# One core, delta-rule attention and two expert layers: beta is applied to the solved values instead of to the keys, with new written-out orders for the attention stage

## What is computed

```
k_n = k / (norm(k) + 1e-06)
for t in range(S):
    y[t]  = q[t] @ state
    v_old = state^T k_n[t]
    state = state + beta[t] * outer(k_n[t], v[t] - v_old)
x = reshape(y)                                   # 3072 x 384
h = x @ w_in;  x = (h * tanh(softplus(h))) @ w_out      # d_ff 2048
P = 8 rounds of row and column normalising of exp(x @ w_gate - max)
out = sum over e of P[:, e] * (relu(x @ w1[e]) @ w2[e]) # 8 experts, 1024 wide
```

## Time and profile before

| | us |
|---|---|
| median of 3 runs | 2375.93 |
| lowest, highest | 2375.30, 2376.21 |
| the profiled execution, its own time | 2375.96 |
| its span, first to last instruction | 2374.0 |
| attention, to the last product of wave 11 on PE | about 403.6 of the span |

### The profile page before, as it was taken

The page is one execution under the profiler, slowest core; times in us unless marked ns, Lnnn a source line. Parts: engine busy times, 40 slices in busy tenths (PEclk is TensorE's granted clock), DMA queues, the critical chain, the costliest instruction groups (busy, mean ns, idle before and its releaser), DMA issues.

```text
span 2374.0 us, 38713 instructions
## 1 busy us (share of the span) xinstructions
PE 2339.5 (99%) x15984; PEld 1962.5 (83%) x15984; DVE 1271.0 (54%) x2322; ACT 848.3 (36%) x1887; POOL 421.5 (18%) x344
## 2 busy tenths in 40 slices
PE   6999999999999999999999999999999999999999
PEld 5899998888888788888888888888888888888887
DVE  6888878977777564433333433434333334334344
ACT  4888887756666311111111111111111111111111
...
GB/s 85 60 58 60 50 34 50 59 1 0 0 0 27 35 1 51 45 14 45 9 49 45 14 45 9 49 45 14 45 9 54 40 14 49 5 54 40 18 35 68
DMA packets 101152, 82.28 MB, mean 35 GB/s; under 512 B 75120, under 2 KB 82032, under 8 KB 99056
## 3 DMA queue, kind: packets, MB, share of 16 engines
...
q10 hardware_dynamic: 144, 0.66, 0.1%
...
## 4 chain that ended last, share of the span: by engine, by line
PE 95%; DVE 2%; POOL 1%; issue 0%; ACT 0%; DMA 0%; DVEq 0%; POOLq 0%
PE ex_h L142 47%; PE ex_y L142 45%; PE ex_logits L142 2%; DVE at_gram L480 1%; DVE at_X L524 1%; PE ex_y L581 0%; PE ex_logits L581 0%; POOL at_NT L388 0%; DVE at_norm L475 0%; POOL at_Z L394 0%; DMA at_k_in<-k 0%; DVE at_R L486 0%; ACT at_Z L443 0%; POOL at_bk L356 0%; POOL at_bk L363 0%
## 5 line engine op out<-in xcount | busy, mean ns | idle before, releaser
L1320 DVE SCALAR_TENSOR_TENSOR ex_r_lo<-ex_h,ex_r_hi 128x512 fp32r<-128x512 f32 x384 | 265.1, 690 | 929.5 <-ACT ex_r_hi L1199 929.1
L1199 ACT ACTIVATE ex_r_hi<-ex_h 128x512 fp32r<-128x512 f32 x384 | 229.8, 598 | 1285.0 <-PE ex_h L142 1285.0
L142 PE MATMUL ex_h<-x_lo,ex_w_hi 128*128 128x512 f32 x1152 | 448.1, 389 | 0.0
L142 PE MATMUL ex_h<-x_hi,ex_w_hi 128*128 128x512 f32 x1152 | 448.1, 389 | 0.0
L142 PE MATMUL ex_y<-ex_r_hi,ex_w_lo 128*128 128x512 f32 x1152 | 448.1, 389 | 0.0
L142 PE MATMUL ex_y<-ex_r_hi,ex_w_hi 128*128 128x512 f32 x1152 | 448.1, 389 | 0.0
L142 PE MATMUL ex_y<-ex_r_lo,ex_w_hi 128*128 128x512 f32 x1152 | 448.1, 389 | 0.0
L142 PE MATMUL ex_h<-x_hi,ex_w_lo 128*128 128x512 f32 x1152 | 448.1, 389 | 0.0
L1149 POOL TENSOR_TENSOR ex_w_lo<-ex_stage,ex_w_hi 128x512 fp32r<-128x512 f32 x90 | 115.7, 1287 | 1675.3 <-ACT ex_w_hi L1181 1637.1
L142 PEld LDWEIGHTS ex_h<-x_hi,ex_w_hi 128*128 128x128 f32 x1152 | 216.2, 188 | 45.0 <-issue 0.2
L142 PEld LDWEIGHTS ex_h<-x_hi,ex_w_lo 128*128 128x128 f32 x1152 | 216.2, 188 | 45.0
...
## 6 DMA issues: line engine op xcount, KB each, us to landing
...
```

What stands on the lines that cost most here:

```text
L142: return nc.tensor.matmul(out, lhsT, rhs, start=start, stop=stop)
L1199: nc.scalar.activation(r[0][:, j, :], h_bank[j][:], ACT.Relu).then_inc(hi_ready, 1)
L1320: nc.vector.scalar_tensor_tensor(out=r[1][:, j, :], in0=h_bank[j][:], scalar=0.0, in1=r[0][:, j, :].bitcast(F32), op0=ALU.max, op1=ALU.sub ...
```

## The change

- No `bk`, `bv`, `kbT`: the keys are scaled by the norm alone. `gram` applies beta to the half that becomes A, row by row, and becomes three instructions: two of 128x128 with beta as scalar (L512) and one of 128x256 (L514). `U` multiplies by beta as it copies. `R` subtracts from the plain values, and in the first chunk there is no `R`: `B2` reads the values as loaded. `inv` loses its product with beta.
- `F1` transposes 4 pairs of heads of `kn` in one step for two groups, so there are 2 steps of 4 transposes per wave instead of 4, and 2 copies on ACT.
- The squares and the scaling of wave 0 are each cut in two halves of 8 heads, `sqh.0` and `knh.1` on POOL, `sqh.1` and `knh.0` on DVE. `NT.0`, `NT.3` and `ZZ.2` of wave 0 move from POOL to DVE.
- POOL clears the state; the masks are loaded by SP in two parts, the first 4 behind the keys of wave 0.
- PE first does 12 products of 128x256 of a cleared tile (`WARM_UP`), whose result is not used.
- New order tables; the head now holds waves 0 and 1, the rounds run for r = 2 to 10, and `h1` (three products of the dense layer) stands behind all attention products in the last table.

The core of the diff (tables cut to a line):

```diff
 ATTENTION_ROUND = {
     "PE": (
-        "T5.0@-1 Z5.1@-1 F1.3:3 T5.2@-1 Z5.0@-1 X5.3@-1 res.1@-1 Z5.2@-1 res.0@-1 T5.3@-1 res.2@-1 corr.1@-1 "
+        "res.1@-1 X5.3@-1 Z5.2@-1 res.0@-1 T5.3@-1 corr.1@-1 res.2@-1 Z5.3@-1 corr.0@-1 F2.3:13 corr.2@-1 H.1 "
...
+FIRST_ROUND = 2
+WARM_UP = 12
...
-        for r in range(1, NW - 1):
+        for r in range(FIRST_ROUND, NW - 1):
...
     def pool_program(pool):
+        nc.gpsimd.memset(state[:], 0.0).then_inc(zeroed, 1)
...
-            if kind == "bk":
-                pool.wait_ge(rbeta, n + 1)
-                scaled_by(bk[w][:, :, 0:D], k_in[w][:], norm[w][:, 4, :])
-            if kind == "bv":
...
+            if kind == "sqh":
+                pool.wait_ge(loaded_k[w], 16 * (c + 1))
+                nc.gpsimd.tensor_tensor(square[:, HALF[g]], k_in[w][:, HALF[g]], k_in[w][:, HALF[g]], ALU.mult).then_inc(squared, 1)
...
+            if kind == "knh":
+                pool.wait_ge(rnorm, n + 1)
+                nc.gpsimd.tensor_tensor(kn[w][:, HALF[g], 0:D], k_in[w][:, HALF[g]], by_norm(n)[:, HALF[g]],
+                                        ALU.mult).then_inc(scaled, 1)
...
     def dve_program(dve, fill):
+        nc.vector.memset(U[0][:], 0.0).then_inc(blank, 1)
...
-                nc.vector.tensor_tensor(norm[w][:, 4, :], norm[w][:, 3, :], beta_of(n), ALU.mult).then_inc(rbeta, 1)
...
-                nc.vector.tensor_tensor(gram[w][g][:, b], O_bank[i][:].rearrange("p (i a t) -> p i a t", i=2, a=2),
-                                        nupper_upper.unsqueeze(2).to_broadcast([P, 2, 2, P]),
-                                        ALU.mult).then_inc(O_drained[i], 1)
+                for a in range(2):
+                    head = 4 * g + 2 * a + b
+                    nc.vector.scalar_tensor_tensor(out=gram[w][g][:, b, 0, a, :], in0=O_bank[i][:, a * P:(a + 1) * P],
+                                                   scalar=beta_of(n)[:, head:head + 1], in1=nupper, op0=ALU.mult, op1=ALU.mult)
+                nc.vector.tensor_tensor(gram[w][g][:, b, 1, :, :], O_bank[i][:, 2 * P:4 * P].rearrange("p (a t) -> p a t", a=2),
+                                        upper.unsqueeze(1).to_broadcast([P, 2, P]), ALU.mult).then_inc(O_drained[i], 1)
...
-                if first_chunk(n):
-                    nc.vector.tensor_copy(R[g][:], bv[w][:, 4 * g:4 * g + 4, :]).then_inc(R_copied[g], 1)
...
-                nc.vector.tensor_copy(U[g][:, :, 0:D], cols4(O_bank[i])).then_inc(O_drained[i], 1)
+                nc.vector.tensor_tensor(U[g][:, :, 0:D], cols4(O_bank[i]),
+                                        beta_of(n)[:, 4 * g:4 * g + 4].unsqueeze(2).to_broadcast([P, 4, D]),
+                                        ALU.mult).then_inc(O_drained[i], 1)
...
     def pe_program(pe, fill):
+        pe.wait_ge(blank, 1)
+        zeros = U[0][:].rearrange("p j e -> p (j e)")
+        for i in range(WARM_UP):
+            mm(nc, O_bank[0][:, 0:2 * P], zeros[:, 0:P], zeros)
...
-                for x, src in enumerate((kn[w], bk[w]) if w else (bk[w], kn[w])):
-                    for a in range(2):
-                        h0 = 4 * g + 2 * a
-                        last = nc.tensor.transpose(O_bank[i][:, (2 * x + a) * P:(2 * x + a + 1) * P],
-                                                   src[:, h0:h0 + 2, :].rearrange("p h d -> p (h d)"), ident)
+                for x in range(4):
+                    h0 = 8 * g + 2 * x
+                    last = nc.tensor.transpose(O_bank[i][:, x * P:(x + 1) * P],
+                                               kn[w][:, h0:h0 + 2, :].rearrange("p h d -> p (h d)"), ident)
```

More of the change, by code:

```diff
@@ L333, in sp_program @@
         load_k(sp, 0)
+        sp.dma_start(mask[:, 0:4], masks[:, 0:4]).then_inc(masks_in, 16)
         sp.dma_start(beta_t[:], beta).then_inc(beta_in, 16)
+        load_q(sp, 0)
         load_k(sp, 1)
-        load_v(sp, 0)
-        load_q(sp, 0)
+        sp.dma_start(mask[:, 4:], masks[:, 4:]).then_inc(merge_masks_in, 16)
         load_q(sp, 1)
+        for n in range(W):
+            load_v(sp, n)
         for kind, g, n in steps("SP"):
-            if kind == "loadv" and n > 0:
-                sp.wait_ge(v_scaled, n)
+            if kind == "loadv" and n >= W:
+                for x in range(G):
+                    if first_chunk(n - W):
+                        filled(sp, "B2", x, n - W)
+                    else:
+                        drained(sp, "B1", x, n - W)
                 load_v(sp, n)
@@ new lines, in step @@
+                nc.vector.tensor_tensor(gram[w][g][:, b, 1, :, :], O_bank[i][:, 2 * P:4 * P].rearrange("p (a t) -> p a t", a=2),
+                                        upper.unsqueeze(1).to_broadcast([P, 2, P]), ALU.mult).then_inc(O_drained[i], 1)
+            elif kind == "NT":
+                for b in range(2):
+                    drained(dve, "F2", g, n, b)
+                nc.vector.tensor_tensor(by_parity(NT[w][g][:]), four22(ident), gram[w][g][:, :, 0, :, :],
+                                        ALU.add).then_inc(NT_ready[g], 1)
+            elif kind == "ZZ":
+                dve.wait_ge(NT_ready[g], n + 1)
+                if n > 0:
+                    dve.wait_ge(M_filled[g], m_count(n - 1, ("Z", 0)))
+                nc.vector.tensor_tensor(Z2[g][:], NT[w][g][:], four(z2mask), ALU.mult).then_inc(Z2_ready[g], 1)
```

134 lines of the change are left out of this document (68 added, 66 removed), and 136 rows, old and new, of tables (ATTENTION_HEAD, ATTENTION_LAST, ATTENTION_ROUND).

## The result

The changed kernel takes 2363.01 us (median of 4 runs, 2362.57 to 2364.76), the kernel before 2376.07 in the same session. The ratio is 0.9948, with a 95% interval of 0.9936 to 0.9961. It is faster by 13 us where 23 were forecast, and it misses the range's end of 2362 by 1 us.

A forecast was written before the change was run, and what follows sets the result against it. The prediction took PE, busy 99% of the span, as the bound. Its terms, 9.5 + 2.5 + 9.8 + 1.2 = 23.0 us, against 2375.96 gave 2353.0 us, with a range from 2345 to 2362.

The forecast's parts named there:

- Start: Up to wave 0's first `H`: halved squares and scaling, shorter queues; 9.5 us gained, bounds 6 and 12.
- the 1.3 assumed: Wave 0's squares in halves on POOL and DVE, one after the other: 1.3 us; lower bound 0.75 if together.
- one of the cases of the forecast: The 12 cleared products at half clock: 12 us from about 1.2 on; counted 0, with 2.5 us as bound.
- Waves 0 and 1: From the first `H` to that of wave 2: less DVE and ACT work gives 2.5 us, bounds 0 and 6.
- the third rival: Cleared products stay at low clock, delay the transposes, and what follows runs at low clock too: 2357 us; chance 0.12.
- A steady round: Eight attention rounds: 0.94 us of transposes and 0.28 of waiting go from each, 30.66 to 29.44; 9.8 us in all.
- Two signs: Signs of a wrong forecast: rounds above 30 us with a PE gap before `X` or `T`; last attention product after 383 us.
- The wait of 0.28 us: PE's one wait in a round, before `F2.0`, behind DVE's 1.03 us norm product; expected to go.
- Grams: Each gram in three DVE pieces in the rounds: 0.74 us against 0.60, adding 8 x 0.14 to DVE.
- The first rival: Something other than PE holds the round; only the start and waves 0 and 1 pay, 12.0 us: 2364; chance 0.08.
- The slower rival: Fixed price per gram piece makes DVE the bound of each round, deciding from 0.45 us per piece: 2426 us; chance 0.02.
- The last round and wave 11: End of attention: the last round loses 1.2 us, wave 11 gives 0 with bounds -2 and +2; 1.2 us.

The follow-up runs named there:

- g2: The changed kernel run again as it is, for comparison: 2362.50 us, ratio 0.9946.
- c1: Changed kernel with ten cleared products instead of twelve and the three `h1` products before the two `W` of wave 11: 2363.51 us, ratio 0.995.
- b2: Kernel before, with only the transposes of `kn` (two of four per `F1` step) and half of ACT's copy: 2374.07 us, round 30.71 us.
- b1: Kernel before, without the norm's product with beta (L475): 2372.27 us, ratio 0.9986, round 30.37 us.
- b5: Kernel before, without the norm's product with beta, with half the transposes and with grams in three pieces: 2385.77 us, round 31.44 us.
- b3: Kernel before, without the norm's product with beta and with half the transposes: 2370.68 us, ratio 0.9981, round 30.37 us.
- a1: Changed kernel with each gram drained by one DVE instruction again, beta left out of the grams: 2355.74 us, round 30.00 us.
- e1: Changed kernel with the squares' sum behind the four `eX3`, ten cleared products, `h1` and `g.1` earlier in wave 11: 2366.04 us, ratio 0.9961.
- f4: f2 with ten cleared products, and `h1` and the first tile's gates before the two `W` of wave 11: 2361.20 us, ratio 0.9939.
- a2: Changed kernel without the DVE step that adds 1e-6 to the norm: 2363.26 us, ratio 0.9947, round 30.40 us.
- f2: Changed kernel with the squares' sum before `eX2.0` and the norm's last two DVE steps before the next round's `U.2`: 2362.46 us, round 30.41 us.

## Why the prediction was wrong

**Start: right**, 10.5 us for 9.5 (9.9 in g2). The changed kernel, POOL and DVE at the start:

```profile
4.15 1.20 POOL L395 TENSOR_TENSOR at_square<-at_k_in 128x384 f32<-128x384 f32 x1 [2.06 <-DMA at_k_in<-k]
7.16 1.20 POOL L404 TENSOR_TENSOR at_kn<-at_k_in,at_norm 128x384 f32<-128x384 f32 x1 [1.81 <-DMA at_k_in<-k]
...
4.10 0.56 DVE L487 TENSOR_TENSOR at_square<-at_k_in 128x384 f32<-128x384 f32 x1 [1.62 <-DMA at_k_in<-k]
5.38 0.95 DVE L490 TENSOR_REDUCE at_norm<-at_square 128x16 f32<-128x768 f32 x1 [0.72 <-POOL at_square L395]
7.11 0.56 DVE L501 TENSOR_TENSOR at_kn<-at_k_in,at_norm 128x384 f32<-128x384 f32 x1
```

The halves go one after the other: POOL's takes 1.20 instead of half of 1.47, longer by most of the 0.56 that DVE takes beside it. From the start of the squares to the end of both is 1.25 us for the 1.3 assumed. That agrees with the rule of the Trainium skill that the prediction cites (SBUF — State Buffer, "Who interferes with whom"). What was not foreseen is that the keys land 1.9 us earlier (4.15 against 6.05 in the earlier trace rows); the masks no longer load beside them, which wasn't tried by itself. Without it the start would have given 8.6 to 9.5, by an estimate from these rows: from the keys' landing to the scaled keys it takes 4.2 us for 4.45 in the forecast, from the transposes to the first `H` 8.25 for 7.5. The early landing was half given back by the cleared products:

```profile
1.17 8.29 PE L160 MATMUL ex_y<-at_U 128*128 128x256 f32 x24 [1.17 <-DVE at_U L476]
9.30 0.60 PE L629 MATMUL ex_y<-at_mask,at_kn 128*128 128x128 f32 x4
```

The passes of the cleared tile stand 0.43 us apart until 6.9 and 0.22 from there, so they began at the lower clock, one of the cases of the forecast. The keys are scaled at 8.36 (7.16 and 1.20), the transposes start at 9.30. c1 has ten cleared products and an equal first `H`, so this 0.9 us is not shown to be worth anything, and "given back" holds for the transposes alone.

**Waves 0 and 1: mis-sized**, 1.4 us for 2.5, inside the bounds. The clock still falls there (0.88 of full speed on average in 17.55 to 45.06, where 28.03 to 57.15 had 0.84 in the earlier trace rows), so the third rival's idle stretches did not cost more than before. How the rest divides between DVE's shorter list and dearer grams was not tried.

**A steady round: the step that failed.** "0.94 us per round, on the path, since nothing else fills a round of PE." It came from busy time and from the absence of a bracket in PE's rows, and both pass over gaps of 0.1 to 0.3 us. b2 took the same work out of the same order and gained 0.01; in its place PE's weight loads wait 0.9 us for three `eX`. Where PE needs a copy that DVE makes of a product issued just before (0.80 us there and back in the window shown), the transposes were what PE did meanwhile. Taken out, they leave the wait. Two signs that the prediction itself had named came true: rounds above 30 us with PE waiting in front of a `T`, and attention's last product later than 383 us (386.1).
- The wait of 0.28 us was right: 0.35 (b1).
- Grams were mis-sized, at 0.74 where they take 0.85. By DVE's share (88% of the round) this looked harmless. In the older order the three pieces cost 1.07 us of a round (b5 against b3), in the new one 0.48 (a1).
- The new order was counted at nothing in the rounds. With the shorter lists of POOL and ACT it recovers 0.96 us (31.44 in b5, 30.48). Without it the rounds would be slower than before.

So, in the order in which the edits were laid on each other, from 30.72: the beta product gives 0.35, the transposes nothing, the pieces take 1.07, the order and what goes with it give 0.96; 30.48. The first rival, something other than PE holding the round, is what happened. Its evidence against, that PE's only gap is 0.28, was the same misreading. It got 0.08. Its 12.0 us for the start and waves 0 and 1 met 11.9; that its 2364 is so near the 2363.0 measured is in part luck, since the rest, to which it gave nothing, came to +1.55, +1.7 and -1.9 and nearly cancelled.

**The slower rival** was nearer than its 0.02: DVE never becomes the busiest engine, and a piece costs 0.26, not 0.45 us. But the pieces do delay PE long before DVE is full. The point from which it decides is not a share of DVE, but a gram later than the product that waits for it.

**Two slips that changed nothing.** ACT and DVE had 4.5 and 4.9 us to spare in a round, not "5 us or more". And the range's lower end of 2345 is 2 us below what its two named terms give (12 + 6 + 9.8 + 1.2 = 29.0, so 2347); it needs the better bound of wave 11 too.

**The last round and wave 11** gave 1.7 us together for 1.2 (-0.8 and +2.5; neither part was tried), and the dense stage gave back 1.9 that I had put at nothing: "the dense and the expert stages shift as a block". With `h1` last, the gates of the first tile come late; PE waits 0.72 us in front of their product; 0.7 us more are lost by the product at 459.45, which waits 0.44 for `x_lo`, and 0.4 only at the very end of the span. e1 and f4 show 0.9 us of it back when `h1` and the gates go first.

**What stays open.** What makes the 0.13 us at `X4.1`; whether a third buffer for the keys would let the transposes fill the gap at `T3.0` (not tried); whether the order or the shorter lists of POOL and ACT make the 0.96 us; why the last round is 0.8 us longer; whether `X2.3` placed earlier would take the wait at `T2.3` away (not tried); and whether 29.4 can be reached at all, since no run has a round below 30.00.

## What to carry to other kernels

Before an operation's time is counted as gained, look at the distance from its start to the start of the next one and at what the next one waits for; if it waits for another engine's answer to something issued earlier, the operation is a filler, and taking it out gains nothing. A busy share is no evidence here, since records of pipelined products overlap and cover the short gaps. The rows of the weight loads are worth a look too: their records are shorter and showed the waits that PE's own rows covered. A fixed order that was made for one set of durations should be made again after each change of them: here the new order and the shorter lists of POOL and ACT were worth 0.96 us a round, and the work taken from PE nothing in the old one.

## What the runs showed beside this

The long time of the product with beta, which the prediction put down to the port that DVE shares with POOL, did not go with that instruction. In the changed kernel the step in front of it, which has one tensor operand, takes as long in most waves:

```profile
L496 DVE TENSOR_SCALAR at_norm<-at_norm x12: 165/822/829, 6.6 to 308.8; 128x16 f32<-128x16 f32 x12
```

The same step took 165/330/803 before, and b1, which has the older order without the product, 165/332/815. Removing it (a2) or moving it (f2) left its neighbours short, so it is this step at this moment that pays; the cause itself was not tried. And a piece of 128 columns out of PSUM, with beta as its scalar, has 338 to 345 ns on average where 0.28 was expected from the rows for 96 and 256 columns; two stand 0.26 apart:

```profile
L512 DVE SCALAR_TENSOR_TENSOR at_gram<-ex_y,at_beta_t,at_mask 128x128 f32<-128x128 f32 x12 | 3.5, 338 | 0.0
```
